# All four low parts of an x block on GpSimd, where VectorE made two of them

## The reference

```
out = softmax(scale * q @ [mem_k, k_ctx].T) @ [mem_v, v_ctx]   # chunks of 32 tokens, 4 x 8 x 768 x 64
h = x @ w_in                                                   # x: 3072 x 512, w_in: 512 x 2048
g = (a0 + a1 h + a2 h^2 + a3 h^3) / (1 + |b0||h| + |b1|h^2 + 1e-6)
x2 = g @ w_out                                                 # w_out: 2048 x 512
a = x2 @ w1 ; b = x2 @ w2 ; y = (a * b) @ w3 @ w_out2          # inner width 1024, result 3072 x 512
```

## Time and profile before

| what | value |
|---|---|
| median of three runs | 1164.13 us |
| the profiled execution | 1163.84 us, its span 1162.1 us |
| PE busy | 1130.8 us, 97% |
| DVE busy | 758.3 us, 65% |
| ACT busy | 634.7 us, 55% |
| POOL busy | 195.2 us, 17% |
| attention | until about 241 us of the span |
| first MLP | about 241 to 768 us |
| second MLP | about 761 us to the end |

### The profile page before, as it was taken

How to read it: one execution, slowest core, us unless ns; L and a number is a source line. 1 busy time by engine, 2 the same in 40 slices (tenths; PEclk the granted TensorE clock), 3 DMA queues, 4 the chain that set the end, 5 groups by cost and what they waited for, 6 DMA issues and landing times.

```text
span 1162.1 us, 16875 instructions
## 1 busy us (share of the span) xinstructions
PE 1130.8 (97%) x5776; PEld 929.7 (80%) x5776; DVE 758.3 (65%) x1223; ACT 634.7 (55%) x1303; POOL 195.2 (17%) x224
## 2 busy tenths in 40 slices
PE   8988999889999999999999999999999999999998
PEld 6876777678878888888888888888888888888886
DVE  4389999969999999999999898841112121111111
ACT  3267888867687687687787787731212222121211
POOL 3525555502212212212210010010000000000000
PEclk9999999999999999999999999999999999999999
DMA  7867888521121121121120025520101002010000
GB/s 262 250 160 191 203 202 209 154 64 55 46 82 54 45 81 54 45 81 54 45 72 0 0 72 217 181 110 1 73 0 36 36 0 72 0 72 0 36 1 37
DMA packets 138161, 97.43 MB, mean 84 GB/s; under 512 B 88976, under 2 KB 117648, under 8 KB 137104
## 3 DMA queue, kind: packets, MB, share of 16 engines
q1 hardware_dynamic: 138128, 97.02, 27.3%
HBM read 65.54 MB, written 31.46 MB: 83 GB/s over the span
## 4 chain that ended last, share of the span: by engine, by line
PE 49%; DVE 24%; issue 4%; ACT 2%; ACTq 0%; DVEq 0%
PE banks L1244 22%; PE banks L1259 11%; PE banks L1228 8%; PE banks L163 8%; DVE nr L1149 5%; DVE nr L1146 4%; DVE nr L1153 4%; DVE g_lo L1158 3%; DVE sq L1129 3%; DVE poly L1136 3%; DVE poly L1139 1%; DVE x_lo L1115 1%; ACT y_sb L1051 1%; ACT habs L1025 0%; ACT sq L1028 0%
## 5 line engine op out<-in xcount | busy, mean ns | idle before, releaser
L1228 PE MATMUL banks<-g_hi,weights 128*128 128x512 f32 x768 | 252.1, 390 | 3.3 <-DVE g_lo L1158 2.9
L163 PE MATMUL banks<-x_hi,weights 128*128 128x512 f32 x768 | 251.7, 390 | 1.9 <-PEq L173 1.9
L1244 PE MATMUL banks<-x_hi,weights 128*128 128x512 f32 x768 | 244.2, 389 | 0.0
L1187 DVE TENSOR_TENSOR nr<-habs,banks 128x512 f32<-128x512 f32 x48 | 33.0, 688 | 256.7 <-ACT habs L1081 256.7
L1228 PEld LDWEIGHTS banks<-g_hi,weights 128*128 128x128 f32 x768 | 144.1, 188 | 35.5 <-DVE g_lo L1158 5.4
L163 PEld LDWEIGHTS banks<-x_hi,weights 128*128 128x128 f32 x768 | 144.6, 188 | 32.3 <-issue 2.4
L1244 PEld LDWEIGHTS banks<-x_hi,weights 128*128 128x128 f32 x768 | 144.1, 188 | 30.0
L1081 ACT ACTIVATE habs<-banks 128x512 f32<-128x512 f32 x48 | 28.6, 596 | 245.2 <-PE banks L1244 245.2
L163 PE MATMUL banks<-x_lo,weights 128*128 128x512 f32 x384 | 149.6, 390 | 0.0
L1228 PE MATMUL banks<-g_lo,weights 128*128 128x512 f32 x384 | 149.5, 389 | 0.0
L1244 PE MATMUL banks<-x_lo,weights 128*128 128x512 f32 x384 | 149.4, 389 | 0.0
(11 more groups left out here) (87 smaller groups left out, 1803.2 us busy)
## 6 DMA issues: line engine op xcount, KB each, us to landing
x_raw<-x_transposed_dram SPq DMA_DIRECT2D x12, 1024.0 KB, 5.3
weights<-second_mlp_weights_dram SPq DMA_DIRECT2D x8, 1536.0 KB, 6.3
second_mlp_weights_dram<-split SPq DMA_DIRECT2D x16, 512.0 KB, 3.0
qk_sb<-in_q SPq DMA_DIRECT2D x24, 256.0 KB, 3.4
qk_sb<-in_k SPq DMA_DIRECT2D x24, 256.0 KB
v_sb<-in_v SPq DMA_DIRECT2D x24, 256.0 KB, 2.9
x_transposed_dram<-y_sb SPq DMA_DIRECT2D x24, 256.0 KB, 3.1
x_transposed_dram<-y_sb SPq DMA_DIRECT2D x6, 1024.0 KB, 4.9
```

The lines of the kernel that those rows point to most:

```text
L163: last = nc.tensor.matmul(bank[m % 4][:, :], slot[:, m, a, cols], x[:, c, :], start=c == 0 and n == 0, stop=c == KC - 1 and n == 2)
L1228: last = nc.tensor.matmul(bank[4 + c][:, :], slot[:, m, a, cols], g[:, m % G_BUFS, :], start=m == 0 and n == 0, stop=m == SLOTS - 1 and n ...
L1244: last = nc.tensor.matmul(bank[2 * (j % 2) + w][:, :], bslot[:, j, 2 + 2 * w + a, cols], x[:, c, :], start=c == 0 and n == 0, stop=c == KC ...
```

## The change

POOL makes the low parts of all four chunks, at every block, in the order 0, 1, 2, 3, each as soon as the high part of its chunk is there. DVE's `x_los` is gone in all three places, and with it DVE's semaphore `x_lo_dve`; `x_chunk_ready` and `x_free` count POOL's semaphore alone. The core of the diff:

```
 def x_chunk_ready(pe, sh, n, c):
-    pe.wait_ge(sh.x_lo_pool if c % 2 else sh.x_lo_dve, n * 2 + c // 2 + 1)
+    pe.wait_ge(sh.x_lo_pool, n * KC + c + 1)
...
             pool.wait_ge(ve_placed, TILES * QUADS)
-            for c in (1, 3):
+            for c in range(KC):
                 pool.wait_ge(x_hi_ready, c + 1)
...
             def x_free(n):
-                sp.wait_ge(x_lo_dve, n * 2 + 2)
-                sp.wait_ge(x_lo_pool, n * 2 + 2)
+                sp.wait_ge(x_lo_pool, n * KC + KC)
...
         @block.gpsimd
         def _(pool):
             def x_los(n):
-                for a, c in enumerate((1, 3)):
+                for c in range(KC):
                     pool.wait_ge(x_hi_ready, n * KC + c + 1)
...
         @block.vector
-            def x_los(n):
-                for c in (0, 2):
-                    dve.wait_ge(x_hi_ready, n * KC + c + 1)
-                    nc.vector.tensor_tensor(out=x_lo[:, c, :], in0=x_raw[:, c, :], in1=f32(x_hi[:, c, :]),
-                                            op=ALU.subtract).then_inc(x_lo_dve, 1)
...
             def step(i, m, last=False):
-                if m == SLOTS - 2:
-                    x_los(i + 1)
...
             def step_b(i, j, last=False):
-                if j == JS - 2 and not last:
-                    x_los(i + NBLK + 1)
```

More of the change, by code:

```diff
@@ L138, in __init__ @@
         self.x_loaded, self.coef_loaded = sem("x_loaded"), sem("coef_loaded")
-        self.x_hi_ready, self.x_lo_dve, self.x_lo_pool = sem("x_hi_ready"), sem("x_lo_dve"), sem("x_lo_pool")
+        self.x_hi_ready, self.x_lo_pool = sem("x_hi_ready"), sem("x_lo_pool")
         self.x_used, self.h_ready = sem("x_used"), sem("h_ready")
@@ L670, in coefficients @@
                     .then_inc(sh.coef_ready, 1)
-            def x_los():
-                dve.wait_ge(raw_split, 2 * EARLY + LATE)
-                for c in (0, 2):
-                    dve.wait_ge(x_hi_ready, c + 1)
-                    nc.vector.tensor_tensor(out=x_lo[:, c, :], in0=x_raw[:, c, :], in1=f32(x_hi[:, c, :]),
-                                            op=ALU.subtract).then_inc(sh.x_lo_dve, 1)
             def tile_step(b, pos, ahead):
@@ L688, in tile_step @@
                     copy_kT(*after(b, pos, 2))
-                elif ahead == 1:
-                    x_los()
                 if ahead >= 1:
@@ L871, in mlps @@
         x_loaded, x_hi_ready, x_used = sh.x_loaded, sh.x_hi_ready, sh.x_used
-        x_lo_dve, x_lo_pool, h_ready = sh.x_lo_dve, sh.x_lo_pool, sh.h_ready
+        x_lo_pool, h_ready = sh.x_lo_pool, sh.h_ready
         wf_stored, xt_stored = sh.wf_stored, sh.xt_stored
```

## The result

| | before | after |
|---|---|---|
| median of 10 runs each | 1163.86 us | 1168.60 us |
| range | 1163.02 to 1164.66 | 1166.07 to 1169.12 |
| ratio, with its 95% interval | | 1.0035 [1.0026, 1.0043] |
| the profiled execution | 1163.84 us, span 1162.1 | 1169.04 us, span 1167.3 |

The change makes the kernel slower by 0.35%, some 4.1 us by the ratio and 4.7 by the medians. The forecast was 3.8 us, as a median 1167.9; that is 4.0 above the median of before in this table, since the prediction started from three runs with 1164.13. The profiled execution is 5.2 us longer than that of before.

What follows compares the result with a forecast made beforehand. DVE bounds the first MLP's first four blocks, then PE alone. Three periods 0.88 us longer (2.64) plus 1.12 for the fourth g_lo(13) give 3.76: 1163.84 to 1167.6, as median 1167.9; range 1165.0 to 1169.6.

Steps and rivals of the forecast that it cites:

- The bound: First MLP: DVE sets the first four blocks' period, about 87.5 us; PE's own pace is 87.04, 0.44 a block to gain.
- The turns: First-MLP boundaries: POOL subtraction ends 1.14 us after DVE's last end, held DVE instruction 0.56 after POOL's; fourth g_lo(13) 1.12 late.
- The tie: Fourth first-MLP boundary: POOL's first subtraction starts 0.05 to 0.14 us ahead of g_lo(13) and so holds it.
- Rival 3: First-MLP boundaries: g_lo(13) wins the tie, PE stalls 0.95 us for chunk 3; 4 x 1.05 = 4.2 us, 1168.3; chance 0.18.
- The period: First MLP: DVE's loop 0.88 us longer in three periods, 2.64, plus 1.12 for the fourth g_lo(13): 3.76 us.
- rival 1: First-MLP boundaries: POOL costs DVE nothing; PE regains 0.84 plus three times 0.44, 2.2 us, giving 1162.0; chance 0.05.
- Rival 2: First-MLP boundaries: four POOL instructions take 0.91 us each from DVE, 3.48 given back; 4 x 0.14 = 0.6, 1164.7; chance 0.10.
- rival 4: First-MLP boundaries: no turns, POOL keeps the ports for all four; 3 x 1.7 + 5.0 = 10.1 us, 1174.2; chance 0.05.
- Elsewhere nothing: Fifth and sixth first-MLP boundaries, second MLP and attention add zero; attention's ends -0.5 and +1.1 us.
- 3.48 us set free: First-MLP boundary: gain offered to DVE by dropping its two x_lo, worth at most 1.45 us.

Runs made afterwards that it cites:

- DVE makes all four: Against the kernel before, DVE makes all four low parts in the first MLP and POOL none; 1162.70 us, ratio 0.9989.
- POOL reads nothing: Against the kernel before, POOL writes zeros to all four low parts in the first MLP instead of subtracting; 1162.33 us, ratio 0.9987.
- POOL behind g_lo(13): Against the kernel before, POOL makes all four low parts in the first MLP, but waits until g_lo(13) is done; 1170.24 us, ratio 1.0056.
- the second MLP alone: Against the kernel before, POOL makes all four low parts at the five boundaries of the second MLP only; 1163.88 us, ratio 0.9999.
- second trace of the changed kernel: The changed kernel run again, unchanged, beside the kernel before; 1168.51 us, ratio 1.0036, profiled execution 1168.59 us.
- attention-only one: Against the kernel before, POOL makes all four low parts of the first block, at the attention's end, only; 1164.40 us, ratio 1.0004.
- first-MLP-only kernel: Against the kernel before, POOL makes all four low parts at the six boundaries of the first MLP only; 1167.71 us, ratio 1.0029.

## Why the prediction was right, step by step

- **The bound.** DVE sets the period in the first four blocks and PE has 0.44 us a block to gain: right. Where DVE gets shorter (DVE makes all four, POOL reads nothing), the two periods between the second and the fourth boundary fall to 87.02 to 87.04 and no further.
- **The turns.** Forecast for the fourth boundary, counted from the start of ACT's high parts: g_lo(13) ends at +2.52, L1129 (now L1112) at +4.27, the Newton steps at +5.97 and +7.67, g_lo(14) starts at +9.76. The trace has +2.53, +4.22, +5.93, +7.62 and +9.71. The two turns read at one piece of weights gave the delays at another place to 0.05 us.
- **The tie** went to POOL, which started 0.03 us ahead; forecast were 0.05 to 0.14. It fell the same way at all six boundaries of the three traces with four subtractions and no added wait. Rival 3 didn't occur. Forcing it (POOL behind g_lo(13)) gave more than its 4.2: 5.2 in the boundaries. There POOL starts 0.17 behind g_lo(13)'s end, when the semaphore is there, and its first subtraction ends some 1.46 behind that end instead of the rival's 1.14.
- **The period** was to grow by 0.88 and grew by 0.81: the 0.05 above and 0.02 of rounding. 3 x 0.81 + 1.12 = 3.55 instead of 3.76. The fourth finish_g(13) begins at 588.82 where about 587.4 was forecast; 1.65 of its lateness lies ahead of the first boundary.
- **Rivals 1, 2 and 4.** POOL does hold DVE, so rival 1 is out; with POOL's reads gone, or its subtractions, the gain that it promised does come, but as -1.3 where it had -2.2: the 0.84 of the first boundary doesn't come back in any kernel (PE waits 0.7 to 0.9 there without a hold), and no x split of the first MLP lies ahead of it. Rival 2's fair swap (+0.6) ignored the order: g_lo(13) held for PE, and DVE waiting for ACT. The measured 3.55 is six times as much. POOL and DVE take turns, so rival 4 is out.
- **Elsewhere nothing**: borne out by the attention and the second MLP alone. One reason was wrong in its detail. In the attention I let POOL's three in a row meet DVE's normalising of six heads; in the trace after it is POOL's fourth that holds the two-head one, 1.30 instead of 0.42, and PE waits 0.92 us for it:

```profile
233.99 1.35 POOL L459 TENSOR_TENSOR x_lo<-x_raw,x_hi 128x512 fp32r<-128x512 f32 x1 [1.36 <-ACT x_hi L536]
...
234.32 1.30 DVE L636 TENSOR_TENSOR own<-probs,rsums 128x256 f32<-128x256 f32 x1
```

  POOL's first three took 3.72 us there, not the 4.7 of the forecast. In the second trace of the changed kernel and in that of the attention-only one the two-head instruction took 0.43, so this comes and goes. Its price in the first trace is at most the 0.23 us by which the first MLP's first matmul is later.
- **What the sum lacked** is the clock. The forecast took PE as running at full clock when it comes back from a wait. In two of three traces with a wait of 1.77 to 1.96 us at the first boundary the clock fell behind it, worth 0.9 us of the total; in none of the seven with a wait of 0.9 or less did it. Each timed run has its mean granted clock on record: 0.993 or 0.994 in nine of the ten first runs of the changed kernel and 0.992 to 0.994 in all seven later ones, against 0.995 to 0.997 in 24 of 25 runs of the kernel before in that later session. So most runs of the changed kernel had more time at the lower clock. Such a mean doesn't say where, and the fastest run, 1166.07 us, has 0.994 too. The medians of the changed kernel are 4.7 and 4.4 above before instead of 3.55, which fits; that of the first-MLP-only kernel, with the same steps there, is 3.55 above, which doesn't ask for it. What the clock adds to the median is open.
- **How close.** The forecast of 3.8 us stands on a mechanism that gives 3.55, and the kernel lost 4.1 by the ratio. The turns were 0.21 us too dear in it, and the clock was not in it. That these two go against each other is luck.

## What to carry to other kernels

Look at both engines' operands before work is moved from VectorE to GpSimd: here, where both read two SBUF operands, each GpSimd subtraction that meets a full VectorE queue takes 0.8 to 1.1 us from it, more than the 0.69 of doing the subtraction there. The version without a GpSimd subtraction in the first MLP is the fastest, by 1.3 us against before (its interval ends just short of no difference) and by 0.5% against the changed kernel. Look at who is released at the same moment: the first GpSimd instruction became ready 0.03 us ahead of the one low part that TensorE was waiting for. And when an engine is freed, read what its next instruction waits for; here, with g_lo(13) free, ScalarE's square came 1.86 us later, so of the 3.48 us set free only 1.45 could have been used.

## What the runs showed of the hardware that I had not expected

- TensorE's granted clock can fall to its lower level (1.2 GHz) after it comes back from a wait and stay there for some 3 to 4 us: between 323 and 327 in one trace, behind 1.77 us of waiting, and some 4 us from about 242 in three traces, behind 1.90 us at the change from attention to MLP. The same waits left it at full clock in other executions, of the same kernel too. A wait of 1.8 us thus cost 0.9 us more than itself in some executions.
- The fall at 242 goes with what the clock did shortly before. In the three traces that have it (mean 0.86 over 238 to 250 us) the mean over 225 to 236 us, in the attention's last tiles, is 0.84; in the other seven it is 0.69 there and 1.00 over 238 to 250. Why is not shown.
- A POOL memset of 128x512 float32 takes 0.53 us, also when it starts under a DVE instruction with two SBUF operands, which keeps its 0.69; a POOL subtraction of that size takes 1.29 alone and, started ahead, holds such an instruction to 1.8.
